# Two scans in place of one scan and a reciprocal of every decay product, in a fused linear-attention and feed-forward kernel

## The reference

```python
for t in range(S):
    cur = np.einsum('bhd,bhe->bhde', u[None] * kt, vt)
    y[:, :, t] = np.einsum('bhd,bhde->bhe', rt, state + cur)
    state = wt[:, :, :, None] * state + np.einsum('bhd,bhe->bhde', kt, vt)
...
g = h * np.clip(h + 3.0, 0.0, 6.0) / 6.0      # block 1: h = x @ w_in, x2 = g @ w_out (2048 wide)
...
return silu(xn @ w_gate) * (xn @ w_val) @ w_out   # block 2: xn = rms-normed x2 (1536 wide)
```

## Time and profile before

| | us |
|---|---|
| median of 3 runs (932.55 to 935.83) | 933.13 |
| the profiled execution, its own time | 935.66 |
| its span, first to last instruction | 933.9 |
| TensorE busy in the span (share) | 921.6 (99%) |
| VectorE busy | 521.3 (56%) |
| ScalarE busy | 361.7 (39%) |
| GpSimd busy | 291.9 (31%) |

### The profile page before, as it was taken

The page is one execution under the profiler, slowest core; times in us unless marked ns, Lnnn a source line. Parts: engine busy times, 40 slices in busy tenths (PEclk is TensorE's granted clock), DMA queues, the critical chain, the costliest instruction groups (busy, mean ns, idle before and its releaser), DMA issues.

```text
span 933.9 us, 17547 instructions
## 1 busy us (share of the span) xinstructions
PE 921.6 (99%) x7064; PEld 772.9 (83%) x7064; DVE 521.3 (56%) x752; ACT 361.7 (39%) x786; POOL 291.9 (31%) x244
## 2 busy tenths in 40 slices
PE   7999999999999999999999999999999999999998
PEld 7899988888888888888888888888888888888886
DVE  6888976566666666315774553553463373363332
ACT  4557454354444445336463123223223223223212
POOL 4789544454454444324351011011011001101000
PEclk9999999999999999999999999999999999999999
DMA  9874442233223231014221010010000001000000
GB/s 255 237 208 129 109 131 60 63 105 86 75 61 107 69 83 51 22 39 135 86 83 45 0 35 34 1 34 34 0 34 35 1 19 50 0 1 34 1 1 34
DMA packets 33008, 60.40 MB, mean 65 GB/s; under 512 B 6112, under 2 KB 19936, under 8 KB 32928
## 3 DMA queue, kind: packets, MB, share of 16 engines
q1 hardware_dynamic: 27104, 50.82, 18.7%
q10 hardware_dynamic: 5824, 8.47, 3.1%
HBM read 47.66 MB, written 9.44 MB: 61 GB/s over the span
## 4 chain that ended last, share of the span: by engine, by line
PE 93%; DVE 4%; issue 1%; DMA 1%; ACT 1%; SPq 1%; DVEq 0%; ACTq 0%
PE acc L1079 34%; PE bank L1050 11%; PE bank L1052 11%; PE bank L1051 11%; PE pair L1050 5%; PE pair L1051 5%; PE pair L1052 5%; DVE ki L731 1%; PE acc L1113 1%; PE pair L1132 1%; PE pair L1189 1%; PE pair L1161 1%; DVE cum L719 1%; PE bank L1068 1%; PE bank L1153 1%
## 5 line engine op out<-in xcount | busy, mean ns | idle before, releaser
L1079 PE MATMUL acc<-gs,w_dn 128*128 128x512 f32 (+1 forms) x1512 | 357.0, 382 | 1.2 <-issue 1.2
L1079 PEld LDWEIGHTS acc<-gs,w_dn 128*128 128x128 f32 x1512 | 272.9, 188 | 55.1 <-issue 1.3
L945 POOL TENSOR_TENSOR gs<-act_g,gs 128x512 fp32r<-128x512 f32 (+1 forms) x96 | 122.1, 1272 | 208.3 <-ACT gs L550 208.2
L1050 PE MATMUL bank<-xs,w_up 128*128 128x512 f32 (+1 forms) x459 | 171.9, 374 | 1.4 <-DVE state L762 1.2
L1052 PE MATMUL bank<-xs,w_up 128*128 128x512 f32 (+1 forms) x459 | 169.1, 368 | 0.0
L1051 PE MATMUL bank<-xs,w_up 128*128 128x512 f32 (+1 forms) x459 | 169.0, 368 | 0.0
L801 DVE SCALAR_TENSOR_TENSOR act_g<-act_u,bank 128x512 f32<-128x512 f32 (+1 forms) x112 | 67.5, 603 | 139.8 <-ACT act_u L542 139.8
L869 DVE TENSOR_TENSOR act_u<-act_u,bank 128x512 f32<-128x512 f32 x72 | 49.5, 688 | 146.8 <-ACT act_u L612 146.8
L542 ACT ACTIVATE act_u<-bank,half 128x512 f32<-128x512 f32 (+1 forms) x112 | 70.0, 625 | 150.8 <-PE bank L1052 139.9
L616 ACT ACTIVATE gs<-act_g 128x512 fp32r<-128x512 f32 x72 | 45.5, 632 | 155.9 <-DVE act_g L875 155.9
L1050 PEld LDWEIGHTS bank<-xs,w_up 128*128 128x128 f32 x459 | 86.4, 188 | 18.0 <-DVE state L762 1.6
(11 more groups left out here) (121 smaller groups left out, 1121.6 us busy)
## 6 DMA issues: line engine op xcount, KB each, us to landing
rkn<-in_rkN SPq DMA_DIRECT2D x22, 384.0 KB, 4.1
rkt<-in_rkT SPq DMA_DIRECT2D x44, 192.0 KB, 3.6
val<-in_valN SPq DMA_DIRECT2D x22, 256.0 KB, 3.0
x<-x_dram SPq DMA_DIRECT2D x6, 768.0 KB, 4.2
dec<-in_decT SPq DMA_DIRECT2D x46, 97.5 KB, 2.3
x_dram<-xo SPq DMA_DIRECT2D x5, 768.0 KB, 4.1
out<-xo SPq DMA_DIRECT2D x5, 768.0 KB, 3.3
raw_dn<-in_w_out SPq DMA_DIRECT2D x14, 192.0 KB, 4.8
```

The costliest lines, as they stand in the source:

```text
L945: pool.tensor_tensor(gs[:, f % GRING, 1, tok], act_g[:, f % 2, tok], gs[:, f % GRING, 0, tok].bitcast(F32), ALU.subtract).then_inc(s_glo, 1)
L1050: pe.matmul(dst, w_hi, x_hi, start=first, stop=False)
L1079: last = pe.matmul(ps_o[m][:, tok], w[:, wp, m * P:(m + 1) * P], gs[:, f % GRING, xp, tok], start=f == 0 and a == 0, stop=f == nf - 1 and ...
```

## The change

The keys are no longer divided by c. A scan that runs backwards over dec gives, for each token, the product of the decays behind it up to the stretch's end (tile suffix; column t of a chunk holds the product from t on, so the keys read it one column further, `after`, and the whole product is column 1, `whole`). r is multiplied by c divided by the whole product: a second scan, forwards and in place over dec, starts each chunk from the reciprocal of the whole product (whole1), of which there are 8 per partition. The scores come out the same. The sums need no decay of their own any more; the state is multiplied by the whole product of the group that will read it, before that group's `across`, also for the first two groups.

In the steps: `prep_suffix` takes the place of prep_scan, `prep_prefix` (small reciprocal and scan) that of the reciprocals in INV2; s_cum now counts prefix scans. Groups 0 and 1 get a scale_state. dec is held until POOL's rd has read it, so its load waits for s_rd and is issued one group later.

```diff
@@ tiles and semaphores @@
-        cum = sa("cum", [P, 2, PAIRS, PB, T1])
+        whole1 = sa("whole1", [P, PAIRS, PB, T1])
+        suffix = sa("suffix", [P, 2, CHUNKS + 2])
...
-        s_cum, s_inv, s_rd, s_ki = (sem(n) for n in ("s_cum", "s_inv", "s_rd", "s_ki"))
+        s_suf, s_inv, s_cum, s_rd, s_ki = (sem(n) for n in ("s_suf", "s_inv", "s_cum", "s_rd", "s_ki"))
...
+        def after(g):
+
+            return suffix[0:DP, slot(g), 2:2 + CHUNKS].rearrange("p (c t) -> p c t", t=T1)[:, :, 0:T]
+
+        def whole(g):
+
+            return suffix[0:DP, slot(g), 0:CHUNKS].rearrange("p (c t) -> p c t", t=T1)[:, :, 1:2]
@@ sync @@
-                need(sp, s_cum, g - 1)
+                need(sp, s_rd, g - 1)
...
                 if phase == INV1:
-                    if g + 5 < GROUPS:
-                        load_dec(g + 5)
                     if g + 4 < GROUPS:
+                        load_dec(g + 4)
                         load_rk(g + 4)
...
-                if s == 1:
+                if s == 2:
                     load_dec(4)
-                if s == 2:
                     load_rk(4)
                     load_rkn(4)
-                if s == 3:
-                    load_dec(5)
@@ scalar @@
-                act.wait_ge(s_cum, g + 1)
-                act.activation(last[0:DP, g % LASTS, :], cum[0:DP, slot(g), :, :, T:T1].rearrange("p a b t -> p (a b t)"),
-                               ACT.Copy).then_inc(s_last, 1)
+                act.wait_ge(s_suf, g + 1)
+                act.activation(last[0:DP, g % LASTS, :].unsqueeze(2), whole(g), ACT.Copy).then_inc(s_last, 1)
...
-            for g in range(2):
-                keep_last(g)
@@ vector @@
-            def prep_scan(g):
+            def prep_suffix(g):
 
                 q = slot(g)
                 landed(dve, ldD, g, 2)
                 need(dve, s_ki, g - 1)
-                need(dve, s_rd, g - 1)
-                need(dve, s_last, g - 1)
+                need(dve, s_last, g - 1 - SETS)
+                backwards = (t.rearrange("p a b t -> p (a b t)")[:, ::-1] for t in (
+                    dec[0:DP, q, :, :, :], first1[0:DP, :, :, :]))
+                dve.tensor_tensor_scan(suffix[0:DP, q, 0:CHUNKS][:, ::-1], *backwards, 1.0,
+                                       ALU.mult, ALU.add).then_inc(s_suf, 1)
+
+            def prep_prefix(g):
+
+                q = slot(g)
+                dve.wait_ge(s_suf, g + 1)
+                need(dve, s_cum, g)
+                dve.reciprocal(whole1[0:DP, :, :, 0:1].rearrange("p a b t -> p (a b) t"), whole(g)).then_inc(s_inv, 1)
+                dve.wait_ge(s_inv, g + 1)
                 dve.tensor_tensor_scan(*(t.rearrange("p a b t -> p (a b t)") for t in (
-                    cum[0:DP, q, :, :, :], dec[0:DP, q, :, :, :], first1[0:DP, :, :, :])), 1.0,
+                    dec[0:DP, q, :, :, :], dec[0:DP, q, :, :, :], whole1[0:DP, :, :, :])), 1.0,
                                        ALU.mult, ALU.add).then_inc(s_cum, 1)
-
-            def prep_inv(g, part):
...
             def prep_k(g):
 
                 q = slot(g)
                 landed(dve, ldR, g, 2)
-                dve.wait_ge(s_inv, PAIRS * (g + 1))
-                dve.tensor_tensor(*(t.rearrange("p a b t -> p (a b t)") for t in (
-                    ki[0:DP, q, :, :, :], rkt[0:DP, q, 1, :, :, :], ki[0:DP, q, :, :, :])), ALU.mult).then_inc(s_ki, 1)
+                dve.wait_ge(s_suf, g + 1)
+                need(dve, p_sc, g - 1)
+                keys_taken(dve, p_kt, g - 2)
+                dve.tensor_tensor(ki[0:DP, q, :, :, :].rearrange("p a b t -> p (a b) t"),
+                                  rkt[0:DP, q, 1, :, :, :].rearrange("p a b t -> p (a b) t"), after(g), ALU.mult).then_inc(s_ki, 1)
...
-                    if is_first(g):
...
-                    else:
-                        dve.tensor_tensor(state[0:DP, k, :, b, :], sums, state[0:DP, k, :, b, :], ALU.add).then_inc(s_state, 1)
+                    dve.tensor_tensor(state[0:DP, k, :, b, :], sums, state[0:DP, k, :, b, :], ALU.add).then_inc(s_state, 1)
 
             def scale_state(g):
 
                 dve.wait_ge(s_state, STATE_INCS * g + 2)
+                dve.wait_ge(s_last, g + 1)
                 old = state[0:DP, g % SETS, :, :, :].rearrange("p a b d -> p (a b) d")
-                dve.tensor_tensor(old, old, last[0:DP, g % LASTS, :].unsqueeze(2).broadcast_to([DP, PAIRS * PB, D]),
+                dve.tensor_tensor(old, old, last[0:DP, (g + SETS) % LASTS, :].unsqueeze(2).broadcast_to([DP, PAIRS * PB, D]),
                                   ALU.mult).then_inc(s_state, 1)
...
                 if phase == INV1 and g + 3 < GROUPS:
-                    prep_scan(g + 3)
-                if phase in (INV1, INV2) and g + 3 < GROUPS:
-                    prep_inv(g + 3, phase - INV1)
+                    prep_suffix(g + 3)
+                if phase == INV2 and g + 3 < GROUPS:
+                    prep_prefix(g + 3)
...
+            dve.memset(suffix[:, :, CHUNKS:CHUNKS + 2], 1.0).then_inc(s_const, 1)
+            dve.memset(whole1[:, :, :, 1:T1], 0.0).then_inc(s_const, 1)
@@ gpsimd, prep_r @@
-                    rd[0:DP, q, :, :, :], rkt[0:DP, q, 0, :, :, :], cum[0:DP, q, :, :, 0:T])), ALU.mult).then_inc(s_rd, 1)
+                    rd[0:DP, q, :, :, :], rkt[0:DP, q, 0, :, :, :], dec[0:DP, q, :, :, 0:T])), ALU.mult).then_inc(s_rd, 1)
```

More of the change, by code:

```diff
@@ L50 @@
 T1 = T + 1
+CHUNKS = PAIRS * PB * T1
 NT = S // T
@@ L123, in build @@
         nt = sb("nt", [P, TT])
-        gap = sb("gap", [P, 1448])
+        gap = sb("gap", [P, 1972])
         raw = sb("raw", [P, SRING, KT * P])
@@ L340, in dec_half @@
         def dec_half(eng, g, j):
-            n = rows_of(g, j)
+            n = D if j else HI2
             eng.dma_start(dec[HI2 * j:HI2 * j + n, slot(g), :, :, :], decT[g // SETS, g % SETS, j, 0:n]).then_inc(ldD[slot(g)], 16)
@@ L716, in prep_scan @@
                 need(dve, s_ki, g - 1)
-                need(dve, s_rd, g - 1)
-                need(dve, s_last, g - 1)
+                need(dve, s_last, g - 1 - SETS)
[9 more added lines that the diff above has]
+                dve.wait_ge(s_inv, g + 1)
                 dve.tensor_tensor_scan(*(t.rearrange("p a b t -> p (a b t)") for t in (
-                    cum[0:DP, q, :, :, :], dec[0:DP, q, :, :, :], first1[0:DP, :, :, :])), 1.0,
+                    dec[0:DP, q, :, :, :], dec[0:DP, q, :, :, :], whole1[0:DP, :, :, :])), 1.0,
                                        ALU.mult, ALU.add).then_inc(s_cum, 1)
-            def prep_inv(g, part):
-                q = slot(g)
-                if part == 0:
-                    dve.wait_ge(s_cum, g + 1)
-                    need(dve, p_sc, g - 1)
-                    keys_taken(dve, p_kt, g - 2)
-                for p in ((0,), (1, 2, 3))[part]:
-                    dve.reciprocal(ki[0:DP, q, p, :, :], cum[0:DP, q, p, :, 1:T1]).then_inc(s_inv, 1)
             def prep_k(g):
@@ L846, in attention @@
                 if phase == PREP:
-                    if has_state(g) and not is_first(g):
+                    if has_state(g):
                         scale_state(g)
@@ L884, in _ @@
             dve.memset(first1[:, :, :, 0:1], 1.0).then_inc(s_first1, 1)
+            dve.memset(suffix[:, :, CHUNKS:CHUNKS + 2], 1.0).then_inc(s_const, 1)
+            dve.memset(whole1[:, :, :, 1:T1], 0.0).then_inc(s_const, 1)
             dve.wait_ge(s_first1, 2)
             dve.tensor_scalar(ones[:, :].rearrange("p (b t) -> p b t", b=PB), first1[:, 0, :, 1:T1], 0.0, 1.0, ALU.mult, ALU.add).then_inc(s_ones, 1)
+            dve.wait_ge(s_const, 2)
             for g in range(2):
-                prep_scan(g)
-                for part in range(2):
-                    prep_inv(g, part)
+                prep_suffix(g)
+                prep_prefix(g)
                 prep_k(g)
@@ L900, in _ @@
                 if f == 0:
-                    prep_scan(2)
-                if f < 2:
-                    prep_inv(2, f)
+                    prep_suffix(2)
+                if f == 1:
+                    prep_prefix(2)
                 if f == 2:
+                    scale_state(0)
                     sum_bonus(2)
@@ L907, in _ @@
                 if f == 3:
-                    prep_scan(3)
+                    prep_suffix(3)
                 for phase, g in half_a.get(f, ()):
                     attention(phase, g, 0)
-                if f in (4, 5):
-                    prep_inv(3, f - 4)
+                if f == 5:
+                    prep_prefix(3)
             run1(1, cycles(1), 1)
```

8 lines of the change are left out of this document (1 added, 7 removed).

## The result

The changed kernel takes 938.22 us (median of 11, 936.62 to 939.67), the kernel before beside it 934.29 us (11 runs, 931.52 to 936.14). The ratio is 1.0042, 95% interval 1.0031 to 1.0053: 0.4% slower, 3.9 us. The forecast was 931.0 us, its range ended at 935.0, and it had the other sign. A result within 0.5%, either way, is what it held for likeliest.

A forecast was written before the change was run, and what follows sets the result against it. The prediction took PE, busy 921.6 of 933.9 us, to bound the kernel. Its terms, +0.3 - 0.7 - 1.7 and 0, gave -2.1 us from the median of 933.13: 931.0 us, range 928.8 to 935.

The forecast's parts named there:

- rival E: Backward scan: not as fast as the forward one, at twice the duration 2.5 us, giving 934.5 us; chance 0.10.
- Term 1: The start: PE's 1.4 us delay is swallowed by its stand until 20.46 us; +0.3 us, bounds -1.2 and +1.4.
- term 4: From 120 us on, and the queues: VectorE's spare time and early requested dec loads cover the change; 0 us.
- Term 2: First slices, 24 to 36 us: VectorE's shorter chain brings the bonus sum sooner; -0.7 us, bounds -1.0 and +0.3.
- Term 3: Half pass, 94 to 120 us: PE's waits behind three reciprocals shrink; -1.7 us, bounds 0 and -2.0.
- C: First half pass, 70 to 95 us: prefix scans wait for POOL, hidden comes later; +2.8, total 935.5 us; chance 0.12.
- B: PE's stalls stay, being ScalarE's and PE's own, or the start takes back the rest; 932.5 to 934 us; chance 0.22.

The follow-up runs named there:

- the repeat of before: The kernel before, unchanged, profiled a second time: 933.27 us in one execution.

## Why the prediction was wrong

**Durations.** A small reciprocal was priced at 0.15 us and took 0.20, the backward scan ran at 1.24 us as the forward one (rival E falls), and a mean scan took 1.46 us (suffix) and 1.57 us (prefix), within the bounds given. The key product alone took 0.67 us (at 12.82 us) against 0.69 before, so the 0.13 us that the prediction worked out from the Trainium skill (Vector Engine (DVE) Microarchitecture Reference, 5.2) do not show. That a negative step was not measured stands in section 5.1 of the same page, not in 5.2. "So two-operand VectorE work waits for POOL's instruction to end" was right but too narrow in two ways: a one-input tensor_scalar waited as well, and the wait does not end with POOL's instruction but can last through several of them (four, 5.21 us; bound given 3.5). The Trainium skill (SBUF — State Buffer, Who interferes with whom) speaks of whole instructions at a time; that the wait can go on from one to the next, these runs show. What ends it they don't: the scan got its turn after four, the scaling after rd and two of three splits, with POOL still at work. VectorE's fall was 7 us short of the forecast: the scans added 35.8 us, within the 30 to 37 given, but the scalings of the state added 4.9 us (18.5 against 13.6) where 1.4 was allowed, and the small reciprocals took 4.8 in place of 3.6.

**Term 1** (+0.3): the chain was right to 0.5 us up to the bonus matmuls (its sum comes to 13.4, not 13.3, with a key product of 0.54 us where the earlier trace rows has 0.69), and the step "if that is what PE stands for, 1.4 us are swallowed" failed. It held the packet's time fixed. The key product's earlier end released SP's weight loads 2.4 us sooner (16.07 to 13.64), and the packet came 2.1 us later. With the loads late again it came 1.7 us sooner, which is one execution. The term was +2.1 at 20.3 us, above its bound of +1.4. The prediction counted the loads of dec under term 4, but not these, which no line of the diff touches. Nor did the clock recover: the earlier trace rows had 0.50 at 22 to 24 us, and after the change it was 0.50 from 18 to 20 and 0.64 over 24 to 28 us, where it had been 0.96:

```profile
24.00:28.00 4.00, 4.00 (x24) 3.79 (x24) 2.04 (x5) 2.12 (x6) 3.74 (x4) 0.64 1.06 299
```

The Trainium skill (Runtime: NRT & Kernel Launch, Instruction fetch mechanics) has the next block of 256 instructions fetched while the one before is executed, and from that the prediction placed the request ahead of the bonus matmuls. The traces agree only so far that the packet can start 0.3 us behind the first of them (13.34 and 13.01 us, the kernel before with early loads). If the request is put 256 instructions back, the time from there to the packet's start is an estimate of 1.3 to 7.9 us over these runs, and that was what mattered.

**Term 2** (-0.7): it came out at +2.2. "Plus up to 0.8 if the scaling waits for POOL" is the mis-sized term: it waited 2.9 us (3.42 against 0.54). It allowed for less than one POOL instruction; rd was held back by the scan itself (idle 2.94 us), so that rd and the splits stood in one run just as the scaling came. With the splits moved the shift at 35.6 us is 2.6 us smaller. A fall of the clock behind PE's stand, which no term had, adds to it: 0.64 from 36 to 40 us in place of 1.00, while the shift grows by 1.3 us from 33.5 to 38 us.

**Term 3** (-1.7): its wait was not a property of the kernel. The earlier trace rows shows it, the repeat of before does not, nor do the two executions with early loads. The first profile is 2.4 us longer than the second, 1.5 us of it between 88.5 and 109.5 us, where the term stood. A gain was forecast on a delay that stood in one execution of four.

**Term 4** (0) held: from 109.5 us on the shift changes by -0.5 us, and no wait for the loads of dec or for the state appears later. Its reason was weaker than it reads: in the earlier trace rows VectorE has 13 us to spare in 40, which is about 6 in a group's cycle of 19 us, not 12.

**Rivals.** C (0.12) was the mechanism of the third step, and the sum had it at nothing: its price, +2.8 with a wait of over 1.3 us, was right in size (2.0 and 2.9 us by the ratios without and with the start mended), though it was priced as three cycles at 70 to 95 us and came mainly as one wait at 62. Its time was low since the start and the first slices were lost beside it. B had the sentence "the start takes back what the rest gives" and was too mild. That 2.1 us are gained when all three are away equals the forecast sum only by accident: that kernel lacks 20 scans and has a better start.

## What to carry to other kernels

Work taken off an engine with slack bought nothing here (37.7 us of VectorE); what the change put in front of others on that engine was its price. Where two engines take turns, allow for several of the neighbour's instructions in a row, not for one of them. Before a stall in a single trace is counted as gain, look whether a second execution has it, and look whether a mending would help the kernel before as well. And whoever moves the end of an instruction should list every queue that waits for its count: here a semaphore paced loads on another engine's queue, and a stall that no edited line touches moved with them.

## What the runs showed of the hardware that was not expected

- A TENSOR_SCALAR of 112x8 with one input took 3.03 us beside a run of GpSimd instructions; the small RECIPROCAL of the same size took 0.20 us with GpSimd quiet (6.16 us) and 0.20 beside its rd (61.98 us).
- One scan (1.24 us alone) took 5.20 to 5.47 us in seven kernels, at the same place, through four GpSimd instructions back to back: VectorE got no turn between them, but did get one ahead of the fifth. Three reciprocals at that place took 2.56 us, as they do alone.
- One instruction packet of 16 KB started at 13.3 to 20.3 us in kernels with nearly the same order of instructions up to there, and at 13.3 and 18.3 us in two executions of one kernel. In the one at 13.3 us PE's clock stayed at 1.00, and it was 3 us shorter than that kernel's median.
